# A first chunk grouped by two batches, and a first step in two half steps of 256 tokens

## Chip, core and metric

The kernel runs on one core of a Trainium2 chip. The metric is the time of one execution on the device, in microseconds (us). The core has five engines that run beside each other and meet at semaphores: TensorE (PE in the rows, its weight loads PEld), VectorE (DVE), ScalarE (ACT), GpSimd (POOL) and SyncE (SP), which issues most DMAs. Each takes its own instructions strictly in order.

## What is computed

A decayed linear attention gives y; y goes through a first two-matrix block with h * cos(h) between, and the result through a second block that takes the maximum of three products.

```python
# q, k, v, alpha: [4 batches, 8 heads, 768 tokens, 48]; alpha between 0.8 and 1
for t in range(768):
    state = alpha[t] * state + outer(k[t], v[t])      # 48 x 48 for each batch and head
    y[t] = q[t] @ state
x = y as [3072 tokens, 384]
h = x @ w_in                  # 384 x 2048
x = (h * cos(h)) @ w_out      # 2048 x 384
h = max(x @ w1, x @ w2, x @ w3)
out = h @ w_out2
```

## The kernel before

**Chunks, groups, units.** The 768 tokens are 6 chunks of 128, for 4 batches: 512 tokens in a chunk (`TOK`). Attention works in units: one unit is two heads of one batch over one chunk, a chunk has 16 (`UNITS`). Four units with the same two heads, one for each batch, are a group. For a group VectorE scans alpha into `decay` (L500, L502, for each unit) and takes `inv_decay` (L516); GpSimd multiplies q and k by them (`mul_decay` L288 and L289, `mul_inverse` L295 and L296); ScalarE copies q into `q_split` (L373, L374). A unit on TensorE is `stage1` (scores and a transpose, L719, L721), then `outputs` (L733, L734, from chunk 1 on also L737) and `increment` (L749); between them VectorE masks the scores (`mask_scores`, L531). The state is brought up to date from the increment: in chunk 0 by a copy on ScalarE (`first_state`, L362), later by VectorE (`new_state`, L541). In chunk 0 the increments lie in banks of their own (`inc_ps0`); later they lie in the score banks, and `stage1` waits for `state_done`. The output y of a group fills one PSUM bank of 512 columns, `y_ps`.

**Splitting.** Products of the two blocks are made of three matmuls with a high and a low part of each operand (`split_mm`, L755 to L757): the high part is a rounding copy on ScalarE, the low part a subtraction on VectorE. So y becomes `x_hi` (L344, L349) and `x_lo` (L546, L551), the weights `w_hi` (L355) and `w_lo` (`low_weights`, L559), g becomes `g_hi` (L395) and `g_lo` (L606).

**The first block's step.** Step c runs chunk c through the first block in 16 tiles of the inner width. A tile is `hidden1` (9 matmuls of 512 columns into one of two `h_ps` banks), later `accumulate1` (9 matmuls into three banks that stay open for all 16 tiles). Between: `turns` on ScalarE (L414: h over 2 pi, plus a quarter), `whole` on VectorE (L622: rounding), `frac` on GpSimd (L318: turns less whole, in the place of turns), `cosine` on ScalarE (L429), `gated` on VectorE (L600: cosine times h, from now on the gate), `g_hi` on ScalarE, `g_lo` on VectorE. `hidden1` of tile i waits for the gate of tile i - 2. Steps 0 to 4 carry the attention of the next chunk, one unit in a tile:

```python
for i in range(TILES1):
    hidden1(c, s, i)
    if i >= 2: accumulate1(c, i - 2)
    if i < last: stage1(c + 1, i + 1)
    outputs(c + 1, i)
    increment(c + 1, i)
```

**The start.** A prelude does the whole attention of chunk 0 before step 0: 16 units, with one weight tile of 16 loaded (SyncE, six stage slots), rounded (ScalarE) and subtracted (VectorE) in each. Steps 0 to 3 are two turns of a hardware loop of two steps; steps 4 and 5, the prelude and parts of the second block are written out. All order is by hand: each engine's queue stands as the code writes it.

## Time and profile before

| | us |
|---|---|
| median of 3 runs | 910.34 (910.02 to 910.39) |
| the profiled execution | 910.33 |
| its span on the core | 908.7 |
| prelude, until step 0's first matmul | 71.9 |
| step 0 | 92.0 |
| steps 1, 2, 3, 4 | 92.0, 92.5, 92.1, 92.4 |
| step 5, without attention | 72.2 |

Over the span PE is busy 95%, DVE 58%, ACT 37%, POOL 21%. The steps' lengths are taken between the copies of the three accumulator banks on ScalarE (L442), step 0's between first matmuls of 512 columns. A row of the profile's lists in order of time gives start, duration, engine, line, operation, what is written and read, shapes and how many; in square brackets how long the engine was idle before it and who ended that. TensorE's durations hold its pipeline's delay, so what matmuls cost one after another is read from their starts.

### The profile page before, as it was taken

What the parts mean: (1) busy time and instruction counts of PE and PEld (TensorE: products, weight loads), DVE (VectorE), ACT (ScalarE), POOL (GpSimd) and SP (SyncE); (2) the same over time, 40 slices, a digit from 0 to 9 for tenths busy, and PEclk for the clock granted to TensorE, in tenths of its full rate; (3) what the DMA queues carried; (4) which work ended last, traced back from release to release, by engine and by line L of the source; (5) the groups of instructions that cost most, each with busy time, mean ns of one, the idle gap of its engine ahead of it and who ended that gap; (6) DMA issues with size and microseconds to landing.
All of it is one profiled execution on the core that took longest, in us unless ns stands there. A gap on an engine that the chain in (4) does not pass through costs nothing.

```text
span 908.7 us, 12980 instructions
## 1 busy us (share of the span) xinstructions
PE 862.0 (95%) x4156; PEld 716.6 (79%) x4156; DVE 527.4 (58%) x1109; ACT 340.6 (37%) x622; POOL 192.3 (21%) x201
## 2 busy tenths in 40 slices
PE   2768999999989999999899999999999999999998
PEld 2557888788878887888788878878888888888887
DVE  7997777687767776777686456643232322323222
ACT  2554444544444444444444455631121212112111
POOL 3232333233323332433233213310000000000000
PEclk9998999999999999999999999999999999999999
DMA  7741011211121112111213002211010000100000
GB/s 206 207 112 40 14 40 40 75 40 40 40 77 40 40 40 74 40 40 40 74 41 117 1 36 64 77 70 35 1 53 18 35 35 35 35 35 0 1 36 35
DMA packets 13772, 47.16 MB, mean 52 GB/s; under 512 B 1968, under 2 KB 2480, under 8 KB 13712
## 3 DMA queue, kind: packets, MB, share of 16 engines
q1 hardware_dynamic: 12992, 42.47, 16.8%
q0 software_dynamic: 720, 3.93, 1.1%
q8 instruction: 32, 0.52, 0.2%
q14 instruction: 28, 0.23, 0.1%
HBM read 36.96 MB, written 9.44 MB: 51 GB/s over the span
## 4 chain that ended last, share of the span: by engine, by line
PE 84%; DVE 5%; DMA 3%; issue 2%; ACT 2%; POOL 2%; SPq 0%; DVEq 0%; ACTq 0%; POOLq 0%
PE h_ps L755 11%; PE h_ps L757 11%; PE h_ps L756 11%; PE acc_pair L755 5%; PE acc_pair L756 5%; PE acc_pair L757 5%; PE score L757 4%; PE score L756 4%; PE score L755 4%; PE score L719 4%; PE acc_last L756 2%; PE acc_last L755 2%; PE acc_last L757 2%; DMA raw<-qka 2%; PE y_ps L733 2%
## 5 line engine op out<-in xcount | busy, mean ns | idle before, releaser
L755 PE MATMUL h_ps<-x_hi,w_hi 128*128 128x512 f32 x450 | 184.8, 411 | 2.8 <-issue 1.6
L318 POOL TENSOR_TENSOR turns<-turns,whole 128x512 f32<-128x512 f32 x90 | 115.3, 1281 | 314.8 <-DVE whole L622 314.8
L757 PE MATMUL h_ps<-x_lo,w_hi 128*128 128x512 f32 x450 | 178.5, 397 | 0.0
L756 PE MATMUL h_ps<-x_hi,w_lo 128*128 128x512 f32 x450 | 178.1, 396 | 0.0
L429 ACT ACTIVATE cosine<-turns 128x512 f32<-128x512 f32 x96 | 60.4, 629 | 155.1 <-POOL turns L318 147.6
L600 DVE TENSOR_TENSOR gated<-cosine,h_ps 128x512 f32<-128x512 f32 x96 | 65.8, 686 | 88.3 <-ACT cosine L429 88.3
L755 PEld LDWEIGHTS h_ps<-x_hi,w_hi 128*128 128x128 f32 x450 | 85.3, 190 | 20.3 <-issue 2.3
L757 PEld LDWEIGHTS h_ps<-x_lo,w_hi 128*128 128x128 f32 x450 | 84.8, 189 | 20.2
L756 PEld LDWEIGHTS h_ps<-x_hi,w_lo 128*128 128x128 f32 x450 | 85.3, 189 | 15.8
L516 DVE RECIPROCAL inv_decay<-decay 112x128 f32<-112x128 f32 x96 | 90.2, 942 | 0.0
L719 PE MATMUL score<-q_split,k_dec 112*128 112x256 f32 x192 | 66.5, 431 | 23.8 <-ACT q_split L374 13.7
L606 DVE TENSOR_TENSOR g_lo<-gated,g_hi 128x512 fp32r<-128x512 f32 x96 | 75.0, 781 | 12.1 <-ACT g_hi L395 10.1
L414 ACT ACTIVATE turns<-h_ps 128x512 f32<-128x512 f32 x96 | 57.0, 594 | 63.7 <-PE h_ps L757 63.6
L462 ACT ACTIVATE g_hi<-gated 128x512 fp32r<-128x512 f32 x36 | 22.8, 632 | 154.5 <-DVE gated L693 154.5
L755 PE MATMUL acc_pair<-g_hi,w_hi 128*128 128x512 f32 x192 | 77.0, 401 | 1.2 <-DVE g_lo L606 1.2
L395 ACT ACTIVATE g_hi<-gated 128x512 fp32r<-128x512 f32 x96 | 60.6, 631 | 46.8 <-DVE gated L600 46.0
L756 PE MATMUL acc_pair<-g_hi,w_lo 128*128 128x512 f32 x192 | 75.9, 395 | 0.0
L757 PE MATMUL acc_pair<-g_lo,w_hi 128*128 128x512 f32 x192 | 75.9, 395 | 0.0
L719 PEld LDWEIGHTS score<-q_split,k_dec 112*128 112x128 f32 x192 | 38.3, 213 | 34.1 <-issue 13.9
L622 DVE TENSOR_SCALAR whole<-turns 128x512 f32<-128x512 f32 x96 | 40.1, 418 | 42.1 <-ACT turns L414 41.5
L756 PE MATMUL score<-x_hi,w_lo 128*128 128x512 f32 x162 | 64.1, 396 | 0.0
L757 PE MATMUL score<-x_lo,w_hi 128*128 128x512 f32 x162 | 64.1, 396 | 0.0
(118 smaller groups left out, 1503.7 us busy)
## 6 DMA issues: line engine op xcount, KB each, us to landing
raw<-qka SPq DMA_DIRECT2D x46, 288.0 KB, 4.8
v_pad<-val SPq DMA_DIRECT2D x24, 288.0 KB, 3.0
block_out<-x SPq DMA_DIRECT2D x6, 768.0 KB, 3.8
x_in<-block_out SPq DMA_DIRECT2D x6, 768.0 KB, 4.3
raw<-wb SPq DMA_DIRECT2D x12, 384.0 KB, 3.1
out<-raw POOLq DMA_DIRECT2D x5, 768.0 KB, 3.5
stage_own<-wa SPq DMA_DIRECT2D x6, 384.0 KB, 4.2
x<-wa SPq DMA_DIRECT2D x6, 384.0 KB, 3.7
```

The source lines that it names most:

```text
L318: nc.gpsimd.tensor_tensor(frac[:], turns[:], whole[:], ALU.subtract).then_inc(S["frac_done"], 1)
L395: nc.scalar.activation(g_hi[:, i % 2], gated[:], ACT.Copy).then_inc(S["ghi_done"], 1)
L414: nc.scalar.activation(turns[:], h_ps[i % 2][:], ACT.Copy, scale=INV_TURN, bias=0.25).then_inc(S["turns_done"], 1)
L429: nc.scalar.activation(cosine[:], frac[:], ACT.Sin, scale=TURN).then_inc(S["cos_done"], 1)
L516: nc.vector.reciprocal(inv_decay[R, s, b], decay[R, s, b]).then_inc(S["inv_done"], 1)
L600: nc.vector.tensor_tensor(gated[:], cosine[:], h_ps[i % 2][:], ALU.mult).then_inc(S["g_done"], 1)
L606: nc.vector.tensor_tensor(g_lo[:, i % 2], gated[:], g_hi[:, i % 2].bitcast(fp32), ALU.subtract).then_inc(S["glo_done"], 1)
L622: nc.vector.tensor_scalar(whole[:], turns[:], ROUND, ROUND, ALU.add, ALU.subtract).then_inc(S["whole_done"], 1)
L719: mm(score[u % 2][:, 0:SCW], k_dec[0:ROWS, p % 2, b], q_split[0:ROWS, p % 2, b], start=True, stop=True)
L755: mm(ps, w_hi[:, w_at], xh, start=first, stop=False)
L756: mm(ps, w_lo[:, w_at], xh, start=False, stop=False)
L757: return mm(ps, w_hi[:, w_at], xl, start=False, stop=final)
```

## The change

- **Chunk 0's groups.** A group of chunk 0 is no longer two heads for four batches, but two batches for four heads (two pairs of heads): its four units are pairs 2(g mod 2) and the next, batches 2(g div 2) and the next (`place0`). The inputs of chunk 0 are laid out so on the host. After two groups, y of two batches, that is of 256 tokens, is whole (all 384 columns of x).
- **Prelude.** It does the first 8 units. Then **half step A** runs the 16 tiles for the first 256 tokens, with 8 units left of chunk 0, one for two tiles. **Half step B** (step 0 of the code, `half` true) runs the 16 tiles for the other 256 tokens with the 16 units of chunk 1. Steps 1 to 5 are as before. Matmuls of the half steps have 256 columns; the number of tiles of 256 is 32, of weights split 16 as before.
- **Buffers of a half step.** turns, whole, cosine and gated hold two half tiles (depth 2), g_hi and g_lo four.
- **GpSimd** does the rounding `whole` of the half steps beside the subtraction, and the low parts of the first six weight tiles; VectorE does the other ten in tiles 0 to 9 of half step A. A semaphore `wlo_pool` counts the six.
- **SyncE** loads three weight tiles ahead of the queries of group 2, and values and weights in another order.
- **Increments of chunk 0** go to the score banks, as later ones do, and `stage1` waits for the state in chunk 0 too.
- **Loops.** The hardware loop over steps 0 to 3 is gone, on all engines; each step is written out.

```diff
@@ over_steps, the tile's slots, the readiness of low weights
+HTOK = TOK // 2
+POOL_W = 6
...
-        def over_steps(eng, body):
-            with eng.Fori(0, (STEPS - 2) // 2) as r:
-                for s in range(2):
-                    body(2 * r + s, s, True, True)
-            body(STEPS - 2, 0, True, False)
-            body(STEPS - 1, 1, False, False)
+        def place0(u):
+            g, e = u // BATCH, u % BATCH
+            return 2 * (g % 2) + e // 2, 2 * (g // 2) + e % 2
+        def slot(t, half):
+            if half:
+                tmp, at = t % 2 * HTOK, t // 2 % 2 * HTOK
+                return h_ps[t % 2][:, 0:HTOK], slice(tmp, tmp + HTOK), (t % 2, slice(at, at + HTOK)), 2, 4
+            return h_ps[t % 2][:], slice(0, TOK), (t % 2, slice(0, TOK)), 1, 2
+        def over_steps(step):
+            step(0, 0, True, True, True)
+            for c in range(1, STEPS):
+                step(c, c % 2, c < STEPS - 1, c < STEPS - 2, False)
+        def low_ready(eng, k):
+            if k < POOL_W:
+                eng.wait_ge(S["wlo_pool"], k + 1)
+            else:
+                eng.wait_ge(S["wlo_done"], k - POOL_W + 1)
@@ GpSimd
+            def low_weights(k):
+                at = slice(k * W1COLS, (k + 1) * W1COLS)
+                pool.wait_ge(S["whi_done"], k + 1)
+                nc.gpsimd.tensor_tensor(w_lo[:, at], stage[k % SLOTS1], w_hi[:, at].bitcast(fp32),
+                                        ALU.subtract).then_inc(S["wlo_pool"], 1)
+            def fraction(t, half):
+                _, cols, _, depth, _ = slot(t, half)
+                if half:
+                    pool.wait_ge(S["turns_done"], t + 1)
+                    wait(pool, "frac_done", t + 1 - depth)
+                    nc.gpsimd.tensor_scalar(whole[:, cols], turns[:, cols], ROUND, ROUND, ALU.add,
+                                            ALU.subtract).then_inc(S["whole_done"], 1)
+                pool.wait_ge(S["whole_done"], t + 1)
+                wait(pool, "cos_done", t + 1 - depth)
+                nc.gpsimd.tensor_tensor(frac[:, cols], turns[:, cols], whole[:, cols],
+                                        ALU.subtract).then_inc(S["frac_done"], 1)
...
-            for g in range(1, PAIRS + 1):
-                decay_qk(g // PAIRS, g % PAIRS)
+            mul_decay(0, 1)
+            low_weights(0)
+            mul_inverse(0, 1)
+            low_weights(1)
+            low_weights(2)
+            mul_decay(0, 2)
+            low_weights(3)
+            mul_inverse(0, 2)
+            low_weights(4)
+            low_weights(5)
+            for i in range(TILES1):
+                if i == 4:
+                    decay_qk(0, 3)
+                if i == 10:
+                    decay_qk(1, 0)
+                fraction(i, True)
@@ ScalarE, half step A
+            for u in range(UNITS // 2):
                 if u:
                     first_state(u - 1)
+                if u == BATCH:
+                    x_high0(0)
+                if u == 3:
+                    split_queries(0, 1)
                 high_weights(u)
+            x_high0(1)
+            first_state(UNITS // 2 - 1)
+            split_queries(0, 2)
+            for i in range(TILES1):
+                if i == UNITS // 2:
+                    x_high0(2)
+                if i and i % 2 == 0:
+                    first_state(UNITS // 2 - 1 + i // 2)
+                if i:
+                    g_high(i - 1, True)
+                turn(i, True)
+                if i == 5:
+                    split_queries(0, 3)
+                if i == 11:
+                    split_queries(1, 0)
+                if i < UNITS // 2:
+                    high_weights(UNITS // 2 + i)
+                cosines(i, True)
+            x_high0(3)
+            g_high(TILES1 - 1, True)
@@ VectorE, half step A
+            ahead0 = {**{i: (0, 3, i) for i in range(4)}, **{i + 6: (1, 0, i) for i in range(4)},
+                      **{i + 12: (1, 1, i) for i in range(3)}}
+            for i in range(TILES1):
+                if i:
+                    gate(i - 1, True)
+                if i % 2:
+                    mask_scores(0, UNITS // 2 + i // 2)
+                if i:
+                    g_low(i - 1, True)
+                if i == UNITS // 2:
+                    x_low0(2)
+                if i in ahead0:
+                    scan(*ahead0[i])
+                    inverse(*ahead0[i], ahead0[i][0] % 2)
+                if POOL_W + i < TILES1:
+                    low_weights(POOL_W + i)
+            gate(TILES1 - 1, True)
+            x_low0(3)
+            g_low(TILES1 - 1, True)
@@ TensorE
-                if not first:
-                    pe.wait_ge(S["state_done"], 2 * (n - 1))
+                wait(pe, "state_done", 2 * (n - 1))
...
-                mm(inc_ps0[s] if first else inc_ps[s], scores[:, s, SCW:ATW], heads, start=True,
+                mm(inc_ps[s], scores[:, s, SCW:ATW], heads, start=True,
                    stop=True).then_inc(S["inc_done"], 1)
...
-            for u in range(UNITS):
-                if u < UNITS - 1:
+            for u in range(UNITS // 2):
+                if u < UNITS // 2 - 1:
                     stage1(0, u + 1)
                 outputs(0, u)
                 increment(0, u)
-            pe.wait_ge(S["state_done"], 2 * UNITS)
+            pe.wait_ge(S["xlo_done"], 2)
+            for i in range(TILES1):
+                hidden1(i, i, 0, first_tokens, True)
+                if i >= 2:
+                    accumulate1(i - 2, i - 2, first_tokens, 0, True)
+                if i % 2 == 0:
+                    stage1(0, UNITS // 2 + i // 2)
+                else:
+                    outputs(0, UNITS // 2 + i // 2)
+                    increment(0, UNITS // 2 + i // 2)
+            accumulate1(TILES1 - 2, TILES1 - 2, first_tokens, 0, True)
             stage1(1, 0)
+            accumulate1(TILES1 - 1, TILES1 - 1, first_tokens, 0, True)
```

**TensorE, start of the first block.** Before, the last unit of the prelude and the first tile of step 0 (tiles of 512 columns):

```order
L733 MATMUL y_ps<-scores,v_pad 96x128
L734 MATMUL y_ps<-scores,v_pad 96x128
L749 MATMUL h_ps<-v_pad,scores 112x96
L719 MATMUL score<-q_split,k_dec 128x256
L721 MATMUL score<-ident,k_dec 128x112
L136 UNCONDITIONAL_BRANCH
L136 ISA
L755 MATMUL h_ps<-x_hi,w_hi 128x512
```

Now the end of a tile of half step A, then the start of the next; the increment goes to a score bank:

```order
L894 MATMUL h_ps<-x_lo,w_hi 128x256
L873 MATMUL y_ps<-scores,v_pad 96x128
L874 MATMUL y_ps<-scores,v_pad 96x128
L886 MATMUL score<-v_pad,scores 112x96
L892 MATMUL h_ps<-x_hi,w_hi 128x256
```

Half a unit stands between the matmuls of a tile, and there is no branch.

**VectorE, chunk 0's units.** Before, one unit of the prelude:

```order
L500 SCALAR_TENSOR_TENSOR decay<-raw,ones 112x63
L502 SCALAR_TENSOR_TENSOR decay<-raw,ones 112x64
L531 TENSOR_TENSOR scores<-score,mask 128x368
L516 RECIPROCAL inv_decay<-decay 112x128
L559 TENSOR_TENSOR w_lo<-x,w_hi 128x768
```

Now a tile of half step A, one of those with everything in it:

```order
L722 TENSOR_TENSOR gated<-cosine,h_ps 128x256
L633 TENSOR_TENSOR scores<-score,mask 128x368
L728 TENSOR_TENSOR g_lo<-gated,g_hi 128x256
L596 SCALAR_TENSOR_TENSOR decay<-raw,ones 112x63
L598 SCALAR_TENSOR_TENSOR decay<-raw,ones 112x64
L612 RECIPROCAL inv_decay<-decay 112x128
L679 TENSOR_TENSOR w_lo<-stage_own,w_hi 128x768
```

The gate and g_lo of the tile before now stand in one queue with the scans and the low weights.

**GpSimd, products and subtractions.** Before, at the start of step 0:

```order
L288 TENSOR_TENSOR q_dec<-raw,decay 112x4x64
L289 TENSOR_TENSOR k_dec<-raw,decay 112x4x64
L295 TENSOR_TENSOR q_dec<-raw,inv_decay 112x4x64
L296 TENSOR_TENSOR k_dec<-raw,inv_decay 112x4x64
L316 ISA
L129 REGISTER_ALU
L318 TENSOR_TENSOR turns<-turns,whole 128x512
```

Now in tile 4 of half step A:

```order
L311 TENSOR_TENSOR q_dec<-raw,decay 112x4x64
L312 TENSOR_TENSOR k_dec<-raw,decay 112x4x64
L318 TENSOR_TENSOR q_dec<-raw,inv_decay 112x4x64
L319 TENSOR_TENSOR k_dec<-raw,inv_decay 112x4x64
L337 TENSOR_SCALAR whole<-turns 128x256
L341 TENSOR_TENSOR turns<-turns,whole 128x256
```

The rounding has come in front of the subtraction, behind the same four products.

## Rows read from the trace of the kernel before

**Rows 1.** The page's first line: the span and the number of instructions.

```profile
span 908.7 us, 12980 instructions
```

**Rows 2.** Stretches (us): length, busy time (instructions) by engine, granted clock, DMA.

```profile
72.00:164.00 92.00, 91.20 (x467) 75.92 (x466) 69.42 (x166) 41.22 (x77) 30.56 (x31) 0.98 0.14 33
...
65.00:71.00 6.00, 1.73 (x7) 1.49 (x8) 5.33 (x9) 4.07 (x10) 0.00 (x0) 0.50 0.51 117
...
75.00:79.00 4.00, 4.00 (x23) 3.11 (x21) 2.76 (x8) 1.50 (x3) 0.84 (x2) 1.00 0.00 0
```

**Rows 3.** In order of time, prelude: TensorE's second unit, a state copy.

```profile
14.89 1.08 PE L719 MATMUL score<-q_split,k_dec 112*128 112x256 f32 x2
...
15.95 0.63 PE L733 MATMUL y_ps<-scores,v_pad 128*96 128x128 f32 x2
...
16.80 0.55 PE L749 MATMUL acc_last<-v_pad,scores 128*112 128x96 f32 x2
...
33.33 0.44 ACT L362 ACTIVATE state<-acc_last 48x48 f32<-48x48 f32 x2 [1.65 <-PE acc_last L749]
```

**Rows 4.** In order of time, TensorE: starts of steps, one unit, neighbouring matmuls.

```profile
71.88 0.78 PE L755 MATMUL h_ps<-x_hi,w_hi 128*128 128x512 f32 x1
...
85.53 0.59 PE L719 MATMUL score<-q_split,k_dec 112*128 112x256 f32 x2
...
87.16 0.39 PE L756 MATMUL h_ps<-x_hi,w_lo 128*128 128x512 f32 x1
87.39 0.40 PE L757 MATMUL h_ps<-x_lo,w_hi 128*128 128x512 f32 x1
...
163.85 0.39 PE L755 MATMUL h_ps<-x_hi,w_hi 128*128 128x512 f32 x1
...
257.65 0.47 PE L755 MATMUL h_ps<-x_hi,w_hi 128*128 128x512 f32 x1 [1.65 <-issue]
...
615.65 0.34 PE L839 MATMUL acc_pair<-w_lo,g_hi 128*128 128x384 f32 x1
615.82 0.33 PE L840 MATMUL acc_pair<-w_hi,g_lo 128*128 128x384 f32 x1
```

**Rows 5.** In order of time, TensorE's weight loads behind a unit.

```profile
86.82 0.19 PEld L755 LDWEIGHTS h_ps<-x_hi,w_hi 128*128 128x128 f32 x1
86.93 0.19 PEld L756 LDWEIGHTS h_ps<-x_hi,w_lo 128*128 128x128 f32 x1
```

**Rows 6.** In order of time, the loop from gate to gate in step 0.

```profile
104.27 0.69 DVE L600 TENSOR_TENSOR gated<-cosine,h_ps 128x512 f32<-128x512 f32 x1 [1.18 <-ACT cosine L429]
...
104.99 0.63 ACT L395 ACTIVATE g_hi<-gated 128x512 fp32r<-128x512 f32 x1 [0.49 <-DVE gated L600]
...
107.27 1.28 POOL L318 TENSOR_TENSOR turns<-turns,whole 128x512 f32<-128x512 f32 x1 [3.69 <-DVE whole L622]
...
108.58 0.63 ACT L429 ACTIVATE cosine<-turns 128x512 f32<-128x512 f32 x1 [0.81 <-POOL turns L318]
...
109.25 0.69 DVE L600 TENSOR_TENSOR gated<-cosine,h_ps 128x512 f32<-128x512 f32 x1 [1.20 <-ACT cosine L429]
```

**Rows 7.** In order of time, prelude: GpSimd and VectorE beside each other.

```profile
35.20 1.55 POOL L295 TENSOR_TENSOR q_dec<-raw,inv_decay 112x256 f32<-112x256 f32 x1
35.21 0.95 DVE L559 TENSOR_TENSOR w_lo<-x_in,w_hi 128x768 fp32r<-128x768 f32 x1
...
36.08 0.82 DVE L500 TENSOR_TENSOR_SCAN decay<-raw,ones 112x63 f32<-112x63 f32 x1
```

**Rows 8.** Groups by shape: count | busy us, mean ns | idle before, releaser.

```profile
L516 DVE RECIPROCAL inv_decay<-decay 112x128 f32<-112x128 f32 x96 | 90.2, 942 | 0.0
L500 DVE TENSOR_TENSOR_SCAN decay<-raw,ones 112x63 f32<-112x63 f32 x96 | 28.9, 301 | 6.2 <-DMA raw<-qka 6.2
...
L288 POOL TENSOR_TENSOR q_dec<-raw,decay 112x256 f32<-112x256 f32 x24 | 17.8, 743 | 76.1 <-DVE decay L502 76.1
L264 POOL TENSOR_SCALAR_AFFINE_SELECT ident<-ident 128x112 f32<-128x112 f32 x1 | 0.3, 279 | 1.8 <-DVE mask L484 1.8
```

More of the change, by code:

```diff
@@ L234, in load_weights2 @@
                 sp.dma_start(stage2[k % SLOTS2], part).then_inc(S[f"stage2_in{k % SLOTS2}"], 16)
-            with sp.Fori(2, STEPS) as a:
+            for a in range(2, STEPS):
                 for p in range(PAIRS):
@@ L590, in _ @@
-            for j in range(KT):
-                x_low_quad(0, j, 0)
-            scan(1, 1, 2)
-            inverse(1, 1, 2, 1)
-            def gate(t, i):
-                dve.wait_ge(S["cos_done"], t + 1)
-                wait(dve, "ghi_done", t)
-                wait(dve, "glo_done", t)
-                nc.vector.tensor_tensor(gated[:], cosine[:], h_ps[i % 2][:], ALU.mult).then_inc(S["g_done"], 1)
-            def g_low(t, i):
+                mask_scores(0, b)
+            for b in range(2, BATCH):
+                inverse(0, 1, b, 0)
@@ new lines, in _, with gate @@
+            for b in range(2, BATCH):
+                mask_scores(0, b)
+            for b in range(BATCH):
+                scan(0, 2, b)
+            for b in range(BATCH):
+                inverse(0, 2, b, 0)
+                mask_scores(0, BATCH + b)
+                if b == 0:
+                    x_low0(0)
+            x_low0(1)
+            def gate(t, half):
+                h, cols, _, depth, _ = slot(t, half)
+                dve.wait_ge(S["cos_done"], t + 1)
+                wait(dve, "ghi_done", t + 1 - depth)
+                wait(dve, "glo_done", t + 1 - depth)
+                nc.vector.tensor_tensor(gated[:, cols], cosine[:, cols], h, ALU.mult).then_inc(S["g_done"], 1)
@@ L636, in step @@
                     if i:
-                        gate(t - 1, i - 1)
+                        gate(t - 1, half)
                     if not attend and i in (1, TILES1 - 1):
@@ L651, in step @@
                         scan(*nxt)
-                    if attend:
+                    if attend and not half:
                         whole_turns()
```

223 lines of the change are left out of this document (127 added, 96 removed).

## The prediction

> **What bounds the kernel now.** I read the engines' busy shares over chosen stretches first, then the order of instructions in time at three places, then the groups of instructions. The span is 908.7 us [rows 1]. It falls into a prelude (all of chunk 0's attention, to 71.9 us), six steps, and the second block. Step 0 runs from 71.88 to 163.85 us, that is 92 us, and TensorE is busy for 91.2 of the 92 us [rows 2, 4]: there TensorE is the bound. The prelude is no TensorE work: its matmuls go at half speed (the two score matmuls 1.08 us, against 0.59 us at 85.53) and wait for VectorE's masks between [rows 3, 4]. So 72 us pass before the first dense matmul. The change can win only there and in step 0; steps 1 to 5 and the second block keep their work. I therefore ask one thing: when does step 1 begin, which is 163.85 us before?
>
> **Part 1, the shorter prelude (8 units).** Its queues are TensorE, ScalarE and VectorE in turn. New: the increment now lands in the score bank, so the score matmuls two units on wait for ScalarE's copy of the state, where two other banks carried it before. From the rows: score and transpose 1.06 us (14.89 to 15.95), the two output matmuls 0.85 (to 16.80), the increment 0.55, then ScalarE's copy, which waits for the increment and takes 0.44, with 0.05 on either side [rows 3]. That makes 3.0 us from one increment's end to the next, and nothing hides it, since the copy ends last. The first increment ends at 17.35 as before (the start work ahead of it is unchanged); seven periods of 3.0 make 38.35; the last has no score and no copy ahead of it, -1.5; one query split, two operations of some 0.63 (the 512-column ScalarE operation of [rows 6]), now stands between two state copies, +1.25; the one y bank has to be read between the two groups, +0.8: 38.9. Then ScalarE writes x_hi in four pieces and VectorE x_lo behind it, 2.1 us. **Half step A starts at 41 us.** Six low weights move to GpSimd: at 1.28 us for 512 columns and 0.74 for 256 [rows 6, 8], 768 columns are 1.82 us by the same line, 11 us in all. They lie in GpSimd's idle time, the last ends near 40 us, just hidden, as an estimate along the order of GpSimd's queue; if they slip, A's first tile slips with them. On SyncE's queue three weight loads now stand ahead of a queries load, and later ones wait on GpSimd's count; the loads come 10 us before their readers, so I cost them at nothing.
>
> **Part 2, half step A: 16 tiles of 256 tokens with 8 units of chunk 0.** TensorE: matmuls of 512 columns follow each other by 0.233 us, those of 384 by 0.173 [rows 4], 0.06 us less for 128 columns; so 256 columns are 0.115 us. The lower end is half of 0.233, the upper one the 0.19 us that a weight load shows [rows 5]. But two such loads start 0.11 us apart [rows 5], so a load does not occupy the array's input for its 0.19; I take 0.115. A tile is 18 x 0.115 = 2.07, plus half a unit of about 1.2 = 2.7 us.
> The Trainium skill (TensorE: Matmul & The Clock Gate, Part 3, The mechanism) says that a weight load overlaps a running matmul only when the row group differs. All loads here use all rows; that rule would add load and matmul up, and the page's 107 ns load on 213 ns would give 320 ns for 512 columns. The row says 0.233, so here the trace disagrees and the rule gets no weight beyond the rival below.
>
> Yet TensorE isn't the bound in A. There is a serial loop from tile to tile: VectorE's gate, ScalarE's g_hi, then (behind it on ScalarE) turns of the next tile, GpSimd's rounding and its subtraction, ScalarE's cosine, the next gate. At 512 columns it closes in 4.98 us (104.27 to 109.25), under TensorE's 5.6 us per tile, and is hidden [rows 6]. At 256: VectorE's 0.69 and 0.95 us for 512 and 768 give 0.43; ScalarE's 0.63 for 512 and 0.22 for 48 (half of 0.44) give 0.40 [rows 3, 6, 7]; the subtraction 0.74 [rows 8]. GpSimd's rounding is new. Bounds: 0.28 us (a one-input operation of 112 columns) to 0.74 (two inputs, 256) [rows 8]; I take 0.45, nearer the one-input row. Handing over costs 0.03 to 0.05 each, and an operation queued behind its own engine's last starts 0.1 early. Sum: 0.46 + 0.30 + 0.46 + 0.50 + 0.77 + 0.45 = **2.9 us**, more than TensorE's 2.7.
> VectorE lengthens seven of the tiles: gate 0.43, the wait for g_hi 0.45 (a mask fits in), g_lo 0.35, two scans 0.38, reciprocal 0.87, low weight 0.87 = 3.4 us [rows 7, 8], so 0.5 x 7 = 3.5. And VectorE and GpSimd hinder each other: a GpSimd product of 0.74 took 1.55 beside a low weight, and the scan behind it 0.82 instead of 0.30 [rows 7, 8]. With 1.2 us of GpSimd work in each tile I charge 0.3 on twelve tiles, 3.5 us. The four-product group of GpSimd (3.0 us) stands twice ahead of a rounding; about 1 us of each shows: 2. One query split beside a high weight, one x_low: 1.
> A: first tile until its gate 4.5 (matmuls at half speed for some 3 us) + 15 x 2.9 = 43.5 + 3.5 + 3.5 + 2 + 1 = 58. Its end gains 1 us: x_lo stands ahead of the last g_lo, and the last accumulation waits for that. **A takes 59 us**, to 100.
> The Trainium skill (GPSIMD Engine Reference, Specifications) names VectorE instructions with two SBUF inputs or in a two-port mode as those that contend with GpSimd. The rows agree (1.55 beside 0.95 us); by it the masks, gates and reciprocals stay free, which is why I don't charge every tile in full.
>
> **Part 3, half step B: the other 256 tokens with 16 units of chunk 1.** TensorE: 2.07 + a unit of 1.40 (85.53 to 87.16, less a matmul) [rows 4] = 3.47 a tile, 55.5 in all, and the 2.5 us that step 0 loses over 16 x (4.2 + 1.4). VectorE was busy 69.42 us in step 0 [rows 2], 4.34 a tile. The rounding (0.42) leaves it and two operations shrink by 0.26 each: 3.4 a tile, as long as TensorE's. The scans, which stood ahead of the rounding, now fall beside GpSimd's subtraction: +0.25. So VectorE paces B at 3.65: 58.4 + 2 = **60.5 us**. B ends at 160.5.
>
> **Part 4, loops written out.** TensorE stood 1.65 us at one loop end (257.65) [rows 4]; the neighbouring steps lose part of it to another wait, so the gain is 0.4 us. New code is longer; the steps already written out show no stall, so nothing is charged.
>
> **Sum.** Step 1 begins at 160.5 instead of 163.85: -3.4, and -0.4: span 904.9. The profiled execution took 910.33 us, 1.6 over its span, and the median is 910.34, so **906.5 us**. What the half steps take from the prelude (31 us) they give back almost wholly (59 + 60.5 against 92).
>
> **Rivals.** (a) *Loops only, no hindrance.* If VectorE and GpSimd seldom meet, A is 4.5 + 43.5 + 3 + 1 = 52 and B is 57.5; step 1 begins at 150.5: 896.5 us. For it: reciprocal and GpSimd's subtraction overlap unharmed in step 0. Against: the widened rows. (b) *Slower: VectorE and GpSimd serialize.* If all 1.2 us of GpSimd's tile work adds to VectorE's queue, the seven full tiles of A are 4.2, the other eight 3.3 (55.8 + 4.5 + 3 + 3 = 66) and B is 4.1 a tile plus 2.5 (68); step 1 begins at 175: 921 us. It turns to a loss from 0.12 us more per tile than I charge (3.8 us over 32 tiles). Half-way to it lies 914. (c) *Weight loads bound 256-column matmuls* at 0.19 us: tiles of 4.0 and 4.8 us, A 68, B 79: about 934. Against it the loads 0.11 us apart. (d) *Clock.* TensorE was granted half the clock from 65 to 75 us, after a stretch in which it was idle most of the time, and the full clock (2.4 GHz) after 3 us of dense matmuls [rows 2]. If the gaps of A (2.7 of 3.4 us busy) are enough to lose it, a tile of A costs 18 x 0.23 + 1.2 = 5.4 us, 86 for 59: up to +27, though at that level it is dense and the clock returns. (e) *Nothing:* each saving is met exactly, within 1.8 us.
>
> **How the numbers follow.** This kernel's measurement tells changes over 0.2% (1.8 us) from none. Chances: forecast 0.45 (903 to 910, of which 0.09 within 0.2%), (a) 0.24, (b) 0.20 (0.04 of it within), (c) and (d) 0.06, (e) 0.05. Faster 0.36 + 0.24 = 0.60, same 0.18, slower 0.22. The range reaches from just under (a) to half-way between the middle and the end of (b): 895 to 917, leaving out a little of (a), the end of (b) and (c), (d).
>
> **What would show it.** First 256-column matmul near 41 us; gates of A 2.9 to 3.5 us apart and B's 3.6; ScalarE's turns waiting for g_hi, not for TensorE; starts of 256-column matmuls 0.115 apart; rounding on GpSimd 0.3 to 0.6; full clock from A's start to the end; step 1's first matmul at 160. Wrong if A's gates follow by TensorE's pace, if the prelude misses 41 us by more than 4, if low weights come late, or if steps 1 to 5 change by more than 1 us each.

## The result and the profile after

The changed kernel takes **932.46 us** (median of 4 runs, 931.27 to 932.95) against 910.31 of the kernel before (4 runs, 910.02 to 910.39): ratio 1.0242, 95% interval 1.0224 to 1.0260. It is 22 us slower, where 4 us less was forecast, and 15 us above the upper end of the range. The profiled execution took 932.04 us, 1.6 over its span.

The stretches of the profile after (as [rows 2]): prelude, half step A, half step B up to the start of step 1.

```profile
span 930.4 us, 12867 instructions
...
0.00:41.89 41.89, 20.39 (x73) 16.37 (x73) 27.03 (x70) 16.53 (x36) 21.97 (x28) 1.00 0.68 186
41.89:117.64 75.75, 53.95 (x363) 49.99 (x364) 47.22 (x97) 32.41 (x84) 43.87 (x40) 0.88 0.23 59
117.64:185.77 68.13, 60.46 (x466) 56.08 (x465) 56.55 (x141) 29.37 (x78) 41.19 (x48) 0.98 0.19 45
```

In order of time, TensorE: the first matmul of A and three neighbours in B, and step 1's first matmul of 512 columns (163.85 in [rows 4]).

```profile
41.89 0.44 PE L892 MATMUL h_ps<-x_hi,w_hi 128*128 128x256 f32 x1 [2.91 <-DVE x_lo L672]
...
130.43 0.28 PE L893 MATMUL h_ps<-x_hi,w_lo 128*128 128x256 f32 x1
130.55 0.28 PE L894 MATMUL h_ps<-x_lo,w_hi 128*128 128x256 f32 x1
130.67 0.28 PE L892 MATMUL h_ps<-x_hi,w_hi 128*128 128x256 f32 x1
...
185.77 0.50 PE L892 MATMUL h_ps<-x_hi,w_hi 128*128 128x512 f32 x1
```

All 22 us lie ahead of step 1: it starts 21.9 us late, and from there to the end of the span the kernel takes 744.6 us (before 744.9). A takes 75.75 us where 59 were forecast, B 68.13 where 60.5 were. TensorE was busy for 54 of A's 76 us: it waits, as the prediction said it would, but for longer.

For what? The waits from A's start to B's end (engine, what, releaser: us in all, times, longest), and the groups of GpSimd's two operations of the loop over the same tiles (count | busy us, mean ns | idle before):

```profile
ACT cosine L459 <- POOL turns L341: 66.6, 32, 3.6
POOL whole L337 <- ACT turns L451: 54.3, 26, 7.3
DVE gated L722 <- ACT cosine L459: 33.7, 27, 4.4
...
L337 POOL TENSOR_SCALAR whole<-turns 128x256 f32<-128x256 f32 x32 | 36.4, 1139 | 54.3 <-ACT turns L451 54.3
...
L341 POOL TENSOR_TENSOR turns<-turns,whole 128x256 f32<-128x256 f32 x32 | 29.0, 907 | 2.7
```

These three waits are the arcs of the serial loop from gate to gate. Nobody waits for a transfer, and for TensorE only ScalarE does, at the first tile of A and at that of B:

```profile
ACT turns L451 <- PE h_ps L894: 5.0, 2, 3.6
PE y_ps L873 <- DVE scores L633: 17.2, 8, 3.9
```

TensorE itself waits in A mostly for VectorE's masks (second row), which stand behind the gate of the tile before in VectorE's queue, and so for the same loop. The new operation in the loop, GpSimd's rounding, takes 1139 ns in the mean, where I charged 450 between bounds of 280 and 740. In order of time, one turn of the loop in A, as [rows 6] but with 256 columns:

```profile
46.91 0.42 DVE L722 TENSOR_TENSOR gated<-cosine,h_ps 128x256 f32<-128x256 f32 x1 [2.91 <-ACT cosine L459]
...
47.37 0.42 ACT L465 ACTIVATE g_hi<-gated 128x256 fp32r<-128x256 f32 x1 [0.49 <-DVE gated L722]
47.69 0.36 ACT L451 ACTIVATE turns<-h_ps 128x256 f32<-128x256 f32 x1
...
48.14 1.16 POOL L337 TENSOR_SCALAR whole<-turns 128x256 f32<-128x256 f32 x1 [1.71 <-ACT turns L451]
49.39 1.77 POOL L341 TENSOR_TENSOR turns<-turns,whole 128x256 f32<-128x256 f32 x1
...
49.68 0.89 DVE L679 TENSOR_TENSOR w_lo<-stage_own,w_hi 128x768 fp32r<-128x768 f32 x1
...
51.20 0.42 ACT L459 ACTIVATE cosine<-turns 128x256 f32<-128x256 f32 x1 [2.40 <-POOL turns L341]
...
51.64 0.42 DVE L722 TENSOR_TENSOR gated<-cosine,h_ps 128x256 f32<-128x256 f32 x1 [1.07 <-ACT cosine L459]
```

4.73 us from gate to gate. Two things are long: the rounding (1.16), and the subtraction, 1.77 us beside VectorE's low weight of 0.89; where VectorE does nothing with two inputs it takes 0.73. The bare turn, without low weight or products, is 3.59 to 3.60 us (gates at 95.24 and 98.83 in A, 131.06 and 134.66 in B).

### The profile page after: what moved, and what is told of

Same layout as the page of the kernel before. It is cut to its first block, busy times and chain, and to the rows that moved or that the text cites. A ratio compares the mean times of both kernels' runs of the same rounds, so it can differ in the third digit from the quotient of the medians.

```text
span 930.4 us, 12867 instructions
## 1 busy us (share of the span) xinstructions
PE 864.6 (93%) x4444; PEld 732.7 (79%) x4444; DVE 526.4 (57%) x1122; ACT 345.9 (37%) x674; POOL 248.7 (27%) x256
## 3 DMA queue, kind: packets, MB, share of 16 engines
q1 hardware_dynamic: 12992, 42.47, 16.7%
## 4 chain that ended last, share of the span: by engine, by line
PE 56%; DVE 2%; DMA 1%; ACT 1%; issue 1%; POOL 0%; SPq 0%; DVEq 0%; ACTq 0%
PE h_ps L892 7%; PE h_ps L894 7%; PE h_ps L893 7%; PE score L894 4%; PE score L893 4%; PE score L892 4%; PE acc_pair L892 2%; PE acc_pair L893 2%; PE acc_pair L894 2%; PE score L859 1%; PE acc_pair L991 1%; PE acc_pair L993 1%; PE acc_pair L992 1%; PE acc_last L893 1%; PE acc_last L894 1%; PE acc_last L892 1%
## 5 line engine op out<-in xcount | busy, mean ns | idle before, releaser
L892 PE MATMUL h_ps<-x_hi,w_hi 128*128 128x512 f32 (+1 forms) x498 | 195.9, 393 | 5.8 <-DVE x_lo L672 2.9
L341 POOL TENSOR_TENSOR turns<-turns,whole 128x512 f32<-128x512 f32 (+1 forms) x107 | 125.2, 1170 | 268.4 <-DVE whole L764 265.7
L894 PE MATMUL h_ps<-x_lo,w_hi 128*128 128x512 f32 (+1 forms) x498 | 187.9, 377 | 0.0
L893 PE MATMUL h_ps<-x_hi,w_lo 128*128 128x512 f32 (+1 forms) x498 | 187.7, 377 | 0.0
L722 DVE TENSOR_TENSOR gated<-cosine,h_ps 128x512 f32<-128x512 f32 (+1 forms) x112 | 68.3, 609 | 105.6 <-ACT cosine L459 105.6
L728 DVE TENSOR_TENSOR g_lo<-gated,g_hi 128x512 fp32r<-128x512 f32 (+1 forms) x112 | 80.9, 722 | 16.1 <-ACT g_hi L465 13.8
L892 PE MATMUL acc_pair<-g_hi,w_hi 128*128 128x512 f32 (+1 forms) x224 | 83.1, 371 | 5.7 <-DVE g_lo L728 5.7
L465 ACT ACTIVATE g_hi<-gated 128x512 fp32r<-128x512 f32 (+1 forms) x112 | 63.8, 570 | 49.5 <-DVE gated L722 48.8
L893 PE MATMUL acc_pair<-g_hi,w_lo 128*128 128x512 f32 (+1 forms) x224 | 81.6, 364 | 0.0
L894 PE MATMUL acc_pair<-g_lo,w_hi 128*128 128x512 f32 (+1 forms) x224 | 81.5, 364 | 0.0
L451 ACT ACTIVATE turns<-h_ps 128x512 f32<-128x512 f32 (+1 forms) x112 | 59.3, 529 | 51.4 <-PE h_ps L894 51.1
```

What stands on the lines that cost most here:

```text
L341: nc.gpsimd.tensor_tensor(frac[:, cols], turns[:, cols], whole[:, cols], ALU.subtract).then_inc(S["frac_done"], 1)
L451: nc.scalar.activation(turns[:, cols], h, ACT.Copy, scale=INV_TURN, bias=0.25).then_inc(S["turns_done"], 1)
L465: nc.scalar.activation(g_hi[:, odd, at], gated[:, cols], ACT.Copy).then_inc(S["ghi_done"], 1)
L722: nc.vector.tensor_tensor(gated[:, cols], cosine[:, cols], h, ALU.mult).then_inc(S["g_done"], 1)
L728: nc.vector.tensor_tensor(g_lo[:, odd, at], gated[:, cols], g_hi[:, odd, at].bitcast(fp32), ALU.subtract).then_inc(S["glo_done"], 1)
L892: mm(ps, w_hi[:, w_at], xh, start=first, stop=False)
```

## The experiments

Theory 1 before the experiments: the price of the rounding on GpSimd is the loss. Rival 1: the half steps lose by collisions of VectorE and GpSimd. Rival 2: splitting into half steps loses anyway, by work that doesn't halve. "Step 1 starts" is the first matmul of 512 columns in the profiled execution.

The prelude took 38.8 us in some profiled executions and 41.9 in others, whatever the edit (last section). So the versions are best compared from A's first matmul to step 1 in the profiled executions; the forecast for it was 119.5 us:

| | A's start to step 1, us |
|---|---|
| changed kernel | 143.9 |
| e1 | 127.2 |
| e2 | 136.1 |
| e3 | 134.3 |
| e5 | 124.9 |
| e6 | 121.8 |
| e7 | 129.8 |
| e9 | 116.1 |
| e10 | 115.2 |

### The rounding back on VectorE (e1)

```diff
@@ GpSimd, fraction
-                    nc.gpsimd.tensor_scalar(whole[:, cols], turns[:, cols], ROUND, ROUND, ALU.add,
-                                            ALU.subtract).then_inc(S["whole_done"], 1)
@@ VectorE, behind g_low of the tile before, in both half steps
+                nc.vector.tensor_scalar(whole[:, cols], turns[:, cols], ROUND, ROUND, ALU.add,
+                                        ALU.subtract).then_inc(S["whole_done"], 1)
```

> The changed kernel with the rounding of both half steps on VectorE, behind g_lo, in place of GpSimd; nothing else differs. Theory 1 (the price of the rounding): GpSimd took 1.07 to 1.16 us for it where 0.45 was charged, in the serial loop from gate to gate, 32 times. Then the loop falls from 3.6 us to about 2.75 in tiles with nothing else, VectorE's queue takes over at 3.6 to 4.0 us a tile, and the time falls by 14 to 22 us, to 910 to 918. Theory 2 (VectorE and GpSimd hinder each other, and the rounding's place does not matter): the subtraction on GpSimd still meets the low weights and scans, VectorE gets 0.3 us more a tile, and the time stays within 6 us of 932.

Measured: 912.67 us (10 runs, 909.92 to 916.75), ratio to before 1.0018, interval 1.0003 to 1.0034: 19.8 us less than the changed kernel, as theory 1 expected. From A's start to step 1, where the prelude has no part, it is 16.7 us less: 12.8 between A's gates, 4.3 between B's. The turn of the loop on ScalarE and VectorE, in A:

```profile
91.57 0.42 DVE L717 TENSOR_TENSOR gated<-cosine,h_ps 128x256 f32<-128x256 f32 x1
...
92.35 0.37 ACT L446 ACTIVATE turns<-h_ps 128x256 f32<-128x256 f32 x1
...
92.81 0.29 DVE L730 TENSOR_SCALAR whole<-turns 128x256 f32<-128x256 f32 x1
...
93.18 0.83 POOL L336 TENSOR_TENSOR turns<-turns,whole 128x256 f32<-128x256 f32 x1 [2.09 <-DVE whole L730]
...
94.50 0.42 DVE L717 TENSOR_TENSOR gated<-cosine,h_ps 128x256 f32<-128x256 f32 x1
```

The bare turn is 2.83 to 3.0 us in place of 3.6. The same operation takes 0.29 us on VectorE and 1.07 on GpSimd. Theory 1 holds for the larger part: 16.7 of the 21.9 us by which step 1 came late. Step 1 still starts 5.2 us later than in the kernel before (169.07 against 163.85). So e1 doesn't reach the forecast's 906.5; the later runs ask why.

### What makes the rounding dear (e2)

```diff
-  nc.gpsimd.tensor_scalar(whole[:, cols], turns[:, cols], ROUND, ROUND, ALU.add, ALU.subtract)
+  nc.gpsimd.tensor_scalar(whole[:, cols], turns[:, cols], 1.0, None, ALU.mult)
```

> The changed kernel with GpSimd's rounding cut to one arithmetic operation (a product with 1, so the fraction is zero and the output is not the reference's); same tile, same place, same waits. If GpSimd's price is by the arithmetic operation, its 256 columns fall from 1.07 us to about 0.6 and the time by 32 x 0.45 = 14 us at most, some 10 to 14. If the price is that of one pass over 256 columns whatever is done, the operation stays at 1.07 us and the time at 932.

Measured: 925.98 us, step 1 starts at 178.01.

```profile
L337 POOL TENSOR_SCALAR whole<-turns 128x256 f32<-128x256 f32 x32 | 29.5, 922 | 54.1 <-ACT turns L450 54.1
```

One arithmetic operation in place of two saves 0.22 us of the mean 1139 ns (7.8 us over 32 tiles at the start of step 1); the pass over 256 columns with one input costs the rest. Both expectations missed: the operation neither fell to 0.6 us nor stayed as it was. Even the cheaper form is above the upper bound that I had taken from a two-input operation.

### Without VectorE's low weights in A (e3)

```diff
+  few = slice(k * W1COLS, k * W1COLS + 8)
-  nc.vector.tensor_tensor(w_lo[:, at], stage[k % SLOTS1], w_hi[:, at].bitcast(fp32), ALU.subtract)
+  nc.vector.tensor_tensor(w_lo[:, few], stage[k % SLOTS1][:, 0:8], w_hi[:, few].bitcast(fp32), ALU.subtract)
@@ TensorE, the product with the low weights
-  mm(ps, w_lo[:, w_at], xh, start=False, stop=False)
+  low = w_hi if w_at.start >= POOL_W * W1COLS else w_lo
+  mm(ps, low[:, w_at], xh, start=False, stop=False)
```

> The changed kernel with VectorE's ten low weights of half step A cut to 8 columns each (the rest of the low parts is left out: the matmuls read the high part there, so their number and time stay). Theory 2 in its full form (the collisions and the queue of VectorE make the loss): the subtraction on GpSimd falls from 1.77 to 0.74 us in ten tiles, gates come 3.6 us apart instead of 4.7, and the time falls by 8 to 12 us, to 920 to 924. Theory 1 alone: the loop through GpSimd stays at 3.6 us and at most 3 us are won.

Measured: 920.06 us. Its prelude was 3 us shorter for a reason of its own (below, on the clock), so the gates are compared: from the first gate of A to the last 66.6 us in the changed kernel, 58.0 here. Full tiles fall from 4.7 to 3.7:

```profile
43.96 0.42 DVE L723 TENSOR_TENSOR gated<-cosine,h_ps 128x256 f32<-128x256 f32 x1 [3.83 <-ACT cosine L459]
...
46.72 0.46 DVE L680 TENSOR_TENSOR w_lo<-stage_own,w_hi 128x8 fp32r<-128x8 f32 x1
47.64 0.42 DVE L723 TENSOR_TENSOR gated<-cosine,h_ps 128x256 f32<-128x256 f32 x1 [0.46 <-ACT cosine L459]
```

The low weights cost 8.6 us in A, by their collision with the loop's subtraction. Here the numbers of theory 2 (rival 1) came, its 8 to 12 us and its gates, and theory 1's "at most 3 us" missed: I had taken the two for exclusive, and both are at work. Without these collisions a bare turn is still 3.6 us and a full tile 3.7, so the loop through GpSimd stays the bound. By the table the rounding (e1) is worth 16.7 us and the low weights 9.6.

### The kernel before, with the rounding on GpSimd in one step (e4)

```diff
@@ GpSimd, ahead of the subtraction of a tile i > 0
+                        if attend and not prepare_next:          # step 4
+                            nc.gpsimd.tensor_scalar(whole[:], turns[:], ROUND, ROUND, ALU.add, ALU.subtract)
@@ VectorE
-                    if attend:
+                    if attend and (i == 0 or prepare_next):
                         whole_turns()
```

> The kernel before with the rounding of 15 tiles of step 4 alone (512 columns) on GpSimd instead of VectorE. Theory 1: the operation takes about 2.1 us, the loop from gate to gate grows from 5.0 us to 5.9 to 6.6 and passes TensorE's 5.6 us, so that step 4 takes 97 to 107 us instead of 92.4 and the kernel 5 to 15 us more. Rival: with 5.6 us of TensorE work in a tile there is room, and step 4 stays within 2 us.

Measured: 919.48 us; that step takes 102.65 us (440.11 to 542.76) in place of 92.4, as theory 1 expected.

```profile
L319 POOL TENSOR_SCALAR whole<-turns 128x512 f32<-128x512 f32 x15 | 30.8, 2053 | 32.5 <-ACT turns L419 32.5
L323 POOL TENSOR_TENSOR turns<-turns,whole 128x512 f32<-128x512 f32 x15 | 19.3, 1290 | 1.3
```

The price shows without any half step. From 1070 ns for 256 columns to 2053 for 512 a column costs 3.84 ns; the subtraction, with two inputs, costs 2.1 (0.74 and 1.28 us). On GpSimd the operation with one input is the dearer one.
The Trainium skill (GPSIMD Engine Reference, 4.1 Engine selection) has one-input elementwise work on GpSimd at roughly line rate. These rows disagree: 1.07 us against 0.29 for 256 columns.

### The two half steps joined (e5)

e1, with the hidden products of B's first tile issued ahead of A's last two output products, and chunk 0's last units two tiles earlier, so that x is whole in time:

```diff
+        start0 = {**{2 * k: UNITS // 2 + k for k in range(6)}, 11: 14, 12: 15}
+        done0 = {**{2 * k + 1: UNITS // 2 + k for k in range(6)}, 12: 14, 13: 15}
...
-            accumulate1(TILES1 - 2, TILES1 - 2, first_tokens, 0, True)
             stage1(1, 0)
-            accumulate1(TILES1 - 1, TILES1 - 1, first_tokens, 0, True)
...
+                    elif half:
+                        accumulate1(TILES1 - 2 + i, TILES1 - 2 + i, first_tokens, 0, True)
```

> The kernel of e1 (rounding of the half steps on VectorE) with the two half steps joined: chunk 0's last units are spread so that the last one's output product stands in tile 13 (it stood in tile 15), the last conversion of x and its low half stand in tile 14, and the second half step's first hidden products are issued before the first half step's last two output products, as inside a half step. In e1 the gate of A's last tile stands at 100.32 and that of B's first at 110.25, 9.93 us for what takes 2.9 to 3.3 us within a half step. Theory 1, my forecast left this out: the join is a drained pipeline, so it is worth 9.9 less one tile interval of about 3.3, less what TensorE's lower clock behind the idle time keeps, 5 to 6.5 us; but the state work of two units moves into tiles 12 to 14 that have room of 0.3 us each, and may take 0.5 to 1 back. Time 906 to 908. Theory 2, the join is bound by work that only moves (VectorE's x_lo, ScalarE's five conversions, the state work): the gap shrinks below 2 us, time 911 or more.

Measured: 910.93 us (10 runs), ratio 1.0008, interval 0.9997 to 1.0018: 1.7 less than e1 by the medians, 2.8 by the profiles (gate 1 of A to step 1 in 119.8 us, e1 122.6). In the changed kernel and in e1 the join took 9.1 and 9.9 us from A's last gate to B's first; here 4.5, so the gap fell by 5.4 us, as theory 1 says. But tile 14 now takes 6.1 us, 3.1 more than in e1: ScalarE's five conversions of x moved into it and stand there ahead of `g_hi`. That part of the join was work that only moves, as theory 2 says, and neither theory's sum came alone.

### GpSimd's products behind the subtraction (e6)

```diff
@@ GpSimd, half step A (in B the same for mul_inverse)
-                if i == 4:
-                    decay_qk(0, 3)
-                if i == 10:
-                    decay_qk(1, 0)
                 fraction(i, True)
+                if i in (4, 10):
+                    mul_decay(i // 10, 3 - i // 10 * 3)
+                if i in (5, 11):
+                    mul_inverse(i // 10, 3 - i // 10 * 3)
@@ VectorE, half step B: half_mid, to_mid and from_mid in tile 2 of four, not in tile 0
+                    if half and i % BATCH == 2:
+                        middles(c + 1 + was // PAIRS, was % PAIRS, (s + 1 + was // PAIRS) % 2)
```

> The kernel of e5 with GpSimd's eight products for the queries and keys put behind the subtraction of their tile and spread over two tiles (0,3 at tiles 4 and 5, 1,0 at tiles 10 and 11, in B the second pair behind the subtraction in place of ahead of it), and in B VectorE's three tiny operations for the states moved two tiles on, off GpSimd's products. Theory 1: a product ahead of the subtraction stands in the loop with its full 1.0 to 1.6 us, and VectorE's tiny operations wait for GpSimd's products (0.51 to 0.79 us each in e1, 0.10 to 0.17 alone). In e1 every fourth tile of B takes 5.44 in place of 3.28, 2.16 more, four times 8.6; the tiles 4 and 9 to 10 of A 0.8 and 1.9 more. I expect these to fall to 0.5 to 1 above the others: 5 to 8 us less than e5, 899 to 903. Theory 2: the products cost the same wherever they stand, since GpSimd and VectorE block each other for all of it: less than 2 us, 904 to 907.

Measured: 908.26 us (10 runs), ratio 0.9977, interval 0.9965 to 0.9990. What it removed, from e1's trace (VectorE and GpSimd in the same four microseconds; alone the three small operations take 0.10 to 0.17 us):

```profile
122.97 0.51 DVE L605 TENSOR_TENSOR half_mid<-raw,decay 112x4 f32<-112x4 f32 x1
...
124.26 0.62 DVE L613 TENSOR_TENSOR to_mid<-half_mid,from_mid 112x4 f32<-112x4 f32 x1
124.81 0.79 DVE L620 COPY from_mid<-decay 112x4 f32<-112x4 f32 x1
...
123.42 0.75 POOL L311 TENSOR_TENSOR q_dec<-raw,decay 112x256 f32<-112x256 f32 x1
124.12 0.75 POOL L312 TENSOR_TENSOR k_dec<-raw,decay 112x256 f32<-112x256 f32 x1
124.83 0.75 POOL L318 TENSOR_TENSOR q_dec<-raw,inv_decay 112x256 f32<-112x256 f32 x1
```

Every fourth tile of B falls from 5.44 to 3.86 us, as theory 1 says, but only 3 us arrive where 5 to 8 were expected, and none of them in B, whose gates span 55.7 us as in e5 (55.6): 1.7 come from A's tiles and 1.6 from the join. In B another wait took the place: two tiles grew from 3.28 to 4.56 and 5.26, because the inputs of the next group were late for VectorE's scans, and the tile that got the three small operations took 3.58 to 3.64 in place of 3.28.

```profile
146.81 0.29 DVE L745 TENSOR_SCALAR whole<-turns 128x256 f32<-128x256 f32 x1
148.03 0.72 DVE L596 TENSOR_TENSOR_SCAN decay<-raw,ones 112x63 f32<-112x63 f32 x1 [0.93 <-DMA raw<-qka]
```

### The subtraction on VectorE too (e7)

```diff
@@ VectorE, behind the rounding of a half tile
+                nc.vector.tensor_tensor(frac[:, cols], turns[:, cols], whole[:, cols], ALU.subtract)
```

> The kernel of e6 with the subtraction of the turns' rounding in the half steps on VectorE too, directly behind the rounding, so that GpSimd does nothing but its products there. Theory 1, the loop through the engines sets the pace: the hand to GpSimd and its 0.73 to 0.77 go, VectorE's 0.28 comes in its place, the collision with the low weights goes from the loop; the tile is then VectorE's own work, some 2.6 to 2.9 us in B and 2.9 to 3.3 in A's full tiles, in place of 3.3 and 3.6. Over 32 tiles 8 to 14 us less than e6: 887 to 895. Theory 2, VectorE is the engine that sets the pace already: it gets 0.28 us more in each of 32 tiles, 9 us more than e6, 908 to 912.

Measured: 920.01 us (4 runs), ratio 1.0086, interval 1.0062 to 1.0110: 11.8 more than e6; from A's start to step 1 it is 8.0 more, where theory 2 expected 9. Theory 1 is refuted for the whole, theory 2 right. The stretch 120 to 140 us in B, for e7 (first) and e9 (second; columns as above):

```profile
120.00:140.00 20.00, 18.75 (x146) 17.12 (x145) 19.15 (x55) 8.60 (x23) 3.52 (x5) 1.00 0.25 59
```

```profile
120.00:140.00 20.00, 20.00 (x167) 19.35 (x166) 19.08 (x61) 10.33 (x27) 8.21 (x11) 1.00 0.28 65
```

In e7 VectorE is busy for 19.15 of 20 us and TensorE has gaps; the tiles take 3.74 to 4.23 us (e9: 3.28 to 3.87). In B the loop had room and VectorE had none: all of the 0.43 us that the subtraction takes there shows in a plain tile (3.28 to 3.74). In A theory 1's mechanism is there where VectorE has little to do: two bare turns fall from 2.89 and 2.83 to 2.80 and 2.47 us.

### The kernel before, loops written out (e8)

```diff
-            with eng.Fori(0, (STEPS - 2) // 2) as r:
-                for s in range(2):
-                    body(2 * r + s, s, True, True)
+            for c in range(STEPS - 2):
+                body(c, c % 2, True, True)
```

> The kernel before with the loops over the steps of the first block and the loads of their inputs written out as straight code, the one part of the change that the later steps see. Theory 1 (the forecast's part 4): the jumps' gap goes, 0.2 to 0.5 us less, ratio 0.9995 to 0.9998. Theory 2: straight code must be loaded in place of the loop's, which costs as much or more: ratio 1.000 to 1.001.

Measured: 910.54 us (11 runs), ratio 1.0000, interval 0.9991 to 1.0009. No gain of 0.4 us can be seen; the interval doesn't exclude one.

### Loads earlier, conversions behind the turns (e9)

```diff
@@ SyncE, steps 0 to 3, behind load_qka(a, p)
-                    load_v(a, p)
+                    if p:
+                        load_v(a, p - 1)
+                    else:
+                        load_v(a - 1, PAIRS - 1)
@@ ScalarE, tile 14 of A: now behind turn(14), ahead of cosines(14)
+                if i == 14:
+                    x_high0(3)
+                    first_state(15)
```

> The kernel of e6 with two waits taken away that its trace shows. First, each load of queries, keys and decays stands one load of values earlier in SyncE's queue: in e6 VectorE's scans at tiles 8 and 12 of B waited 0.51 and 0.93 us for the inputs, and the tiles took 4.56 and 5.26 us, since a load of values that waits for four units stood ahead of them. Second, in A's tile 14 ScalarE's five conversions of x stand behind the turns in place of ahead of g_hi, and the scan and reciprocal of that tile move to tile 15: that tile takes 6.11 us in e6. Theory 1: the two tiles of B fall to 3.9 to 4.2, 1.7 us less; A's tile 14 falls to 4.5 to 5, 1.2 to 1.6 less; 905 to 906. Theory 2, the time is VectorE's work, which is only moved: less than 1 us, 907.5 to 908.5.

Measured: **907.14 us** (7 runs, 904.78 to 908.62), ratio 0.9959, interval 0.9944 to 0.9973. Tile 14 falls from 6.1 to 3.5 us, the two late tiles of B to 3.28, and from A's start to step 1 it takes 5.7 us less than e6, where 2.9 to 3.3 were expected. The time of the whole falls by only 1.1 by the medians and misses the expected 905 to 906: this profiled execution has the long prelude, and one later step took 94.7 us for 92.2. Such a step stands in the profiles of e2, e7 and e10 too, each time another one; its cause stays open. The version is 0.4% faster than the kernel before. It comes near the forecast's 906.5, but that is no support for the forecast: it has the rounding in its old place and four repairs that the forecast didn't have. Half steps A and B of it, to hold against those of the changed kernel above:

```profile
41.90:97.00 55.10, 46.51 (x345) 44.15 (x346) 43.36 (x101) 30.57 (x80) 18.78 (x23) 0.97 0.33 83
97.00:157.99 60.99, 59.31 (x484) 56.57 (x483) 57.98 (x168) 31.28 (x83) 25.28 (x33) 1.00 0.19 45
```

### What holds a tile of B (e10)

```diff
-  nc.vector.reciprocal(inv_decay[R, s, b], decay[R, s, b])
+  nc.vector.reciprocal(inv_decay[R, s, b, 0:8], decay[R, s, b, 0:8])     # half step B alone
```

> The kernel of e9 with VectorE's reciprocal of the second half step (B) cut from 128 columns to 8, so 120 of 128 columns of the inverse decay are left as they were: work is left out. It tells what holds a plain tile of B at 3.28 us. Theory 1, VectorE: it is busy without a gap in e6's plain tiles (gate, score mask, two state sums, g_lo, rounding, two scans, reciprocal: 3.28 us from gate to gate, the reciprocal 0.95 of it), so the tile falls until the next limit, the loop's 2.8 to 3.0 us of A's empty tiles or TensorE's 3.2: 0.1 to 0.5 us a tile, 2 to 7 us in B. Theory 2, the loop or TensorE holds it at 3.28 as well: the plain tiles stay within 0.05 us of 3.28.

Measured: 904.03 us in one run; by the profiles from B's first matmul to step 1 60.1 us against e9's 61.0.

```profile
110.00:140.00 30.00, 30.00 (x251) 29.05 (x250) 23.88 (x88) 15.76 (x40) 12.77 (x17) 1.00 0.30 70
```

VectorE falls from 28.7 us busy in these 30 (e9) to 23.9, yet the plain tiles of 3.28 fall nowhere below 3.26 us, and three of them grow to 3.35 to 3.50; those of 3.58 to 3.64 fall to 3.25 to 3.35. In e9 VectorE's gate waits for nobody in B; here it waits for the cosine 13 times, and ScalarE's turns wait for TensorE 8 times. So theory 2 holds for the plain tile: VectorE filled it in e9, and TensorE stood right behind. Taking a quarter of VectorE's work away gives B 0.9 us of 61.

## Why the prediction was wrong

**The step that failed is the term for GpSimd's rounding in Part 2**, "Bounds: 0.28 us (a one-input operation of 112 columns) to 0.74 (two inputs, 256); I take 0.45". It measured 1.07 alone and 1.14 in the mean. Both bounds were wrong: the lower row was a selection over less than half the columns, and the upper rested on an assumption that no row showed, that an operation with one input can't be dearer than one with two. With 1.07 in its place the loop's own sum gives 2.9 + 0.62 = 3.52 us; measured are 3.60. So the mechanism, a serial loop that TensorE waits for, was right, and the size of this term is the largest part of the miss: 0.7 us x 15 turns is 10.5 of the 16.8 us that A took over its forecast. It isn't all of it. Step 1 was forecast for 160.5 and came at 185.8; with the rounding on VectorE (e1) it comes at 169.1, still a small loss to 163.85. The other terms that failed are the collisions, the join and the products in B.

The rest, term by term:
- **Prelude, 41 us:** 41.89 measured. Right within 1 us for this execution; others of nearly the same code have 38.8, which the sum at half speed doesn't foresee (last section).
- **Matmuls of 256 columns, 0.115 us:** 0.117 (130.43, 130.55, 130.67). Right. Rival (c) is refuted, though its 934 is the number nearest to the result, which is luck: its mechanism would show as 0.19 between starts.
- **A's full tiles and collisions:** charged 10 us over the bare loop between first and last gate (3.5, 3.5, 2, 1), measured 66.6 - 15 x 3.60 = 12.6. A low weight beside the subtraction costs about 1 us in a tile, not 0.3 + 0.5; e3 gives 8.6 us for the ten. The mechanism of rival (b) is there, but it is the smaller part.
- **A's ends:** 4.5 us ahead of the first gate and 1 behind the last were charged; measured are 5.0 and 4.1 (last gate 113.50, B at 117.64). The join was priced as if the work went on through it, while no product of B is issued ahead of A's last: 3.1 us too little. With 10.5 for the rounding, 2.6 for the collisions and 0.5 ahead of the first gate this makes up A's 16.8.
- **B, 3.65 us a tile:** the plain tile took 3.60, but not for VectorE's work, as I had it; GpSimd's loop set it, and with the rounding on VectorE it is 3.28. Two tiles in four took 4.17 and 4.60, since the four products stand in the loop: 1.6 us, three times, and 1.2 in the first tile (4.83). These 5.9 us, less 0.8 for the plain tiles, and 2.6 us more at B's ends make up the 7.6 over the forecast.
- **Steps 1 to 5 and the written-out loops:** 0.3 us less between the profiles, within what two executions differ by; e8 shows nothing beyond 0.1%.
- **Clock:** 0.88 in A, where TensorE idled for 22 of 76 us; in the stretch 69 to 73 it is 0.53. I had expected the full clock, rival (d) up to 27 us for its loss. ScalarE, which takes up what TensorE makes, waited for it at the first tiles of A and B alone, so the slow matmuls cost little elsewhere; what they cost at the join no run separates.

```profile
69.00:73.00 4.00, 4.00 (x20) 3.97 (x20) 1.64 (x5) 2.83 (x7) 2.07 (x3) 0.53 0.03 6
...
116.27 0.39 PE L892 MATMUL acc_pair<-g_hi,w_hi 128*128 128x256 f32 x1 [2.99 <-DVE g_lo L728]
...
117.64 0.41 PE L892 MATMUL h_ps<-x_hi,w_hi 128*128 128x256 f32 x1
117.86 0.42 PE L893 MATMUL h_ps<-x_hi,w_lo 128*128 128x256 f32 x1
118.07 0.41 PE L894 MATMUL h_ps<-x_lo,w_hi 128*128 128x256 f32 x1
```

Behind 2.99 us of idle TensorE the matmuls at the join follow each other by 0.21 us, nearly twice the 0.117.

**Where the expected gain went.** A starts 30 us earlier than step 0 did. e9, without the waits found here, spends 55.1 + 61.0 = 116.1 us on the half steps, where step 0 took 92: 24 of the 30 go to the split itself and to the 8 units that moved into A. TensorE is busy for 59.3 of B's 61.0 us, so little is left there. What remains is 5.9 us at the start of step 1, 3.3 by the spans and 3.8 by the medians. The rounding on GpSimd alone costs some three times 5.9 (16.7 us, e1).

## What to carry to other kernels

When a kernel's work is cut into smaller tiles, look for the serial loop from tile to tile first: its handovers don't shrink with the tile (4.98 us a turn at 512 columns, 2.9 at 256 in e1, where TensorE's work halves), and an operation that was hidden at 512 columns is in the open at 256. Before moving an elementwise operation to another engine, find the price of that very operation there, or bound it well above the nearest row; here moving it off a busy engine cost more than it brought, since it stands in the loop. And what frees one wait lets the next engine in the queue show itself (e5 to e6 to e9): read the trace after every repair.

## What the runs showed of the hardware

- GpSimd's one-input tensor_scalar in fp32: 1.07 us for 256 columns, 2.05 for 512 (3.84 ns a column), 0.85 with one arithmetic operation in place of two; VectorE's 0.29. Its two-input tensor_tensor is cheaper, 0.73 and 1.28 us.
- A GpSimd subtraction of 0.73 us took 1.77 beside a VectorE subtraction of 0.89: the longer is about the sum of both. The Trainium skill (SBUF — State Buffer, Who interferes with whom) says that of two such operations one blocks for the whole of the other; the rows agree. By that page the one that issues first goes first, and there the rows disagree: the subtraction, recorded from 49.39, is the one that waits for the low weight, recorded from 49.68, and so in four more tiles of A. It says further that an operation of VectorE with one input from SBUF doesn't contend. `from_mid`, a copy of one input, took 0.79 us beside products and 0.16 alone; whether by the two-port mode that the page excepts, no run here tells.
- The prelude has two lengths. In the profiled executions of e3, e5, e6 and e10 A starts at 38.8 us, in those of the changed kernel, e1, e2, e7 and e9 at 41.9. The same matmuls, e5's (first) and e1's:

```profile
17.98 0.67 PE L866 MATMUL score<-q_split,k_dec 112*128 112x256 f32 x2 [0.62 <-ACT state L415]
```

```profile
17.98 1.19 PE L864 MATMUL score<-q_split,k_dec 112*128 112x256 f32 x2 [0.61 <-ACT state L411]
```

They start at the same time behind the same wait; the first takes about what such a pair takes at full clock (0.59 at 85.53 in [rows 4]), the second nearly twice as much. The granted clock needs care here. Two stretches of e5, then one of e1:

```profile
17.00:24.00 7.00, 3.95 (x26) 3.14 (x25) 5.38 (x8) 5.01 (x11) 4.96 (x4) 1.00 0.93 291
25.00:36.00 11.00, 9.16 (x33) 7.36 (x33) 5.96 (x11) 5.04 (x12) 7.22 (x7) 0.50 0.34 111
```

```profile
13.00:36.00 23.00, 17.38 (x59) 13.72 (x60) 13.76 (x30) 10.56 (x23) 12.30 (x12) 1.00 0.67 187
```

In e5 column and durations agree: 1.00 with 0.67 us, then 0.50 with 1.19 us (25.30). In e1 the column reads 1.00 beside 1.19 us throughout, so ahead of A it can't be taken for the clock, and the durations decide: e5 has the full level of 2.4 GHz for three units and then 1.2, e1 has 1.2 all along. Which prelude an execution had is seen only where it was profiled, but it would account for e1's times, which spread more (909.9 to 916.8) than those of the kernel before beside it (909.5 to 912.1). What decides between the two stays open.
